# Moving the x2 low-part subtraction from GpSimd to VectorE, with a two-step longer lag

## The reference

```python
kv_pool = kv.reshape(B, H//4, 4, W//4, 4, C).mean(axis=(2, 4))      # 768 keys
k = v = kv_pool.reshape(B, -1, C) @ w_sr
x = softmax(q @ k.T / sqrt(C)) @ v                                  # attention

g = relu(x @ w_in) ** 2                                             # first MoE block, d_ff = 2048
x = g @ w_out

h = x @ w_in                                                        # second block
P = a[0] + a[1]*h + a[2]*h**2 + a[3]*h**3
Q = 1 + abs(b[0])*abs(h) + abs(b[1])*h**2
out = (P / (Q + 1e-6)) @ w_out
```

## Time and profile before

| what | value |
|---|---|
| median of 3 runs | 1538.09 us (1538.04 to 1538.12) |
| the profiled execution's own time | 1538.09 us |
| its span (first to last instruction) | 1536.2 us |
| TensorE busy | 1486.7 us, 97% |
| VectorE busy | 1441.0 us, 94% |
| ScalarE busy | 1376.9 us, 90% |
| GpSimd busy | 1186.1 us, 77% |
| mean granted TensorE clock | 0.996 of full |

### The profile page before, as it was taken

One profiled execution on the slowest core, in us unless ns is written; L12 is line 12 of the kernel. 1 busy time (PEld: TensorE's weight loads), 2 busy tenths in 40 slices (PEclk: granted clock), 3 DMA queues, 4 the chain that ended last, 5 costly groups with the idle time before them and its releaser, 6 DMA issues.

```text
span 1536.2 us, 20302 instructions
## 1 busy us (share of the span) xinstructions
PE 1486.7 (97%) x5452; PEld 966.8 (63%) x5452; DVE 1441.0 (94%) x2543; ACT 1376.9 (90%) x2605; POOL 1186.1 (77%) x1167
## 2 busy tenths in 40 slices
PE   5999999999999999999999999999999999999975
PEld 3899999755666556656656665665665665566532
DVE  7888888539999999999999999999999999999998
ACT  3777777679999999999999999999999999999985
POOL 2544444478898888888888989888988988898874
PEclk9999999999999999999999999999999999999998
DMA  6000003000000000000000000000000000000000
GB/s 220 27 22 22 26 20 109 0 0 1 8 7 8 1 8 7 8 7 1 8 8 7 1 8 8 7 1 7 8 8 7 1 8 7 7 1 8 7 7 7
DMA packets 11223, 24.39 MB, mean 16 GB/s; under 512 B 1408, under 2 KB 1536, under 8 KB 10880
## 3 DMA queue, kind: packets, MB, share of 16 engines
q1 hardware_dynamic: 11136, 23.40, 4.5%
HBM read 17.11 MB, written 6.29 MB: 15 GB/s over the span
## 4 chain that ended last, share of the span: by engine, by line
PE 80%; DVE 14%; issue 3%; ACT 1%; POOL 1%; DMA 1%; SPq 0%; POOLq 0%; ACTq 0%; DVEq 0%
PE psum L644 18%; PE psum L633 17%; PE psum L534 10%; PE psum L535 9%; PE psum L536 9%; PE psum L594 6%; PE psum L569 6%; PE psum L580 4%; DVE tb L524 3%; DVE tb L501 3%; DVE tb L507 3%; DVE psum L512 3%; DMA X<-kvT 1%; SPq L186 0%; POOL pnorm L240 0%
## 5 line engine op out<-in xcount | busy, mean ns | idle before, releaser
L292 POOL TENSOR_TENSOR wb<-wb,ub 128x512 f32<-128x512 f32 x384 | 496.6, 1293 | 32.0
L633 PE MATMUL psum<-tb,wout 128*128 128x512 f32 x768 | 396.0, 597 | 5.9 <-DVE tb L524 4.4
L644 PE MATMUL psum<-g,wout 128*128 128x512 f32 x768 | 392.6, 593 | 1.9 <-ACT x2f L380 1.0
L290 POOL TENSOR_SCALAR wb<-ub,babs 128x512 f32<-128x512 f32 x384 | 297.3, 774 | 118.0 <-ACT ub L391 118.0
L392 ACT ACTIVATE tb<-psum,ca 128x512 f32<-128x512 f32 x384 | 311.0, 810 | 0.0
L534 PE MATMUL psum<-x2h,win2h 128*128 128x512 f32 x384 | 291.4, 759 | 18.1 <-DVE tb L524 15.2
L518 DVE TENSOR_TENSOR tb<-tb,psum 128x512 f32<-128x512 f32 x384 | 260.2, 678 | 38.1 <-ACT tb L392 38.1
L501 DVE SCALAR_TENSOR_TENSOR tb<-tb,ca,psum 128x512 f32<-128x512 f32 x384 | 282.6, 736 | 1.4 <-ACT psum L413 0.8
L507 DVE SCALAR_TENSOR_TENSOR tb<-tb,ca,psum 128x512 f32<-128x512 f32 x384 | 283.5, 738 | 0.0
L512 DVE SCALAR_TENSOR_TENSOR psum<-wb,psum 128x512 f32<-128x512 f32 x384 | 263.1, 685 | 0.0
L524 DVE SCALAR_TENSOR_TENSOR tb<-psum,tb 128x512 f32<-128x512 f32 x384 | 261.4, 681 | 0.2
(11 more groups left out here) (65 smaller groups left out, 2257.6 us busy)
## 6 DMA issues: line engine op xcount, KB each, us to landing
qraw<-qT SPq DMA_DIRECT2D x25, 256.0 KB, 2.7
X<-kvT SPq DMA_DIRECT2D x16, 384.0 KB, 8.1
outT<-osb SPq DMA_DIRECT2D x24, 256.0 KB, 2.0
wraw<-w_in SPq DMA_DIRECT2D x2, 1024.0 KB, 10.8
wsr<-w_sr SPq DMA_DIRECT2D x1, 64.0 KB, 1.9
wout<-w_out SPq DMA_DIRECT2D x2, 0.5 KB, 8.1
ca<-coef_a SPq DMA_DIRECT2D x1, 2.0 KB, 2.2
cb<-coef_b SPq DMA_DIRECT2D x1, 1.0 KB, 2.1
```

The lines of the kernel that those rows point to most:

```text
L290: nc.gpsimd.tensor_scalar(w, u, babs[:, 1:2], babs[:, 0:1], ALU.mult, ALU.add).then_inc(v_rdy, 1)
L292: nc.gpsimd.tensor_tensor(w, w, u, ALU.mult).then_inc(w_rdy, 1)
L633: mm(ACC2, wout2[:, f, :], tb[:, t % T_RING, :], start=(f == 0), stop=(f == NF - 1))\
L644: mm(ACC1, wout1[:, f, :], g1[:, t % G_RING, :], start=(f == 0), stop=(f == NF - 1))\
```

## The change

- The copy x2f, its buffer and its semaphore go. GpSimd's subtraction goes.
- VectorE subtracts x2h straight from ACC1 to give x2l, as the first thing in its step 16c + 18, in front of that step's five operations. It waits for x2h_rdy.
- TensorE's first ACC1 matmul of the next chunk now waits for x2_rdy (x2l is there).
- LAG is NF + 5 in place of NF + 3: the second block follows two steps later, and the loop has two steps more.
- On TensorE ACC1 comes before ACC2 within a step. On ScalarE the x2h copy comes before osb, and the square of an even slice is issued one step later (t = s - 2).

```diff
-    LAG = NF + 3
+    LAG = NF + 5
@@ GpSimd
-                t = s - 3
-                if chunk_end(t):
-                    c = t // NF
-                    pool.wait_ge(x2h_rdy, c + 1)
-                    pool.wait_ge(x2f_rdy, c + 1)
-                    nc.gpsimd.tensor_tensor(x2l[:, c % 2, :], x2f[:, c % 2, :], x2h[:, c % 2, :].bitcast(F32),
-                                            ALU.subtract).then_inc(x2_rdy, 1)
@@ ScalarE
+                t = s - 3
+                if chunk_end(t):
+                    c = t // NF
+                    act.wait_ge(g1_used, t + 1)
+                    need(act, h2_rdy, (c - 1) * NF)
+                    nc.scalar.activation(x2h[:, c % 2, :], ACC1, ACT.Identity).then_inc(x2h_rdy, 1)
+
                 t = s - LAG - 5
                 if chunk_end(t):
                     ...
                     nc.scalar.activation(osb[:, c % 2, :], ACC2, ACT.Copy, scale=-1.0).then_inc(o_rdy, 1)
 
-                t = s - 3
-                if chunk_end(t):
-                    c = t // NF
-                    act.wait_ge(g1_used, t + 1)
-                    need(act, h2_rdy, (c - 1) * NF)
-                    nc.scalar.activation(x2h[:, c % 2, :], ACC1, ACT.Identity).then_inc(x2h_rdy, 1)
-                    need(act, x2_rdy, c - 1)
-                    nc.scalar.activation(x2f[:, c % 2, :], ACC1, ACT.Identity).then_inc(x2f_rdy, 1)
-
-                t = s - 1
+                t = s - 2
                 if in_b(t) and on_act(t):
@@ VectorE
             for s in range(STEPS):
+                t = s - 3
+                if chunk_end(t):
+                    c = t // NF
+                    dve.wait_ge(x2h_rdy, c + 1)
+                    nc.vector.tensor_tensor(x2l[:, c % 2, :], ACC1, x2h[:, c % 2, :].bitcast(F32),
+                                            ALU.subtract).then_inc(x2_rdy, 1)
+
                 t = s - LAG - 2
@@ TensorE
+                t = s - 2
+                if in_b(t):
+                    f = t % NF
+                    if t == 0:
+                        pe.wait_ge(x_rdy, NCH)
+                    if f == 0:
+                        need(pe, x2_rdy, t // NF)
+                    pe.wait_ge(sqa_rdy if on_act(t) else sqp_rdy, t // 2 + 1)
+                    mm(ACC1, wout1[:, f, :], g1[:, t % G_RING, :], start=(f == 0), stop=(f == NF - 1))\
+                        .then_inc(g1_used, 1)
+
                 t = s - LAG - 4
                 ...
-                t = s - 2
-                if in_b(t):
-                    ...
-                    if f == 0:
-                        need(pe, x2f_rdy, t // NF)
-                    ...
```

More of the change, by code:

```diff
@@ L104, in build_program @@
         osb = sb("osb", [P, 2, T], F32, atB)
-        x2f = sb("x2f", [P, 2, T], F32, atB)
         psum = ctx.enter_context(nc.psum_tensor("psum", [P, 8, BANK], F32))
@@ L138, in build_program @@
             sem, ("t1_rdy", "t2_rdy", "t3_rdy", "y_rdy", "e_rdy", "g2_rdy", "g2_used", "o_rdy"))
-        x2f_rdy = sem("x2f_rdy")
         o_out = [sem("o_out0"), sem("o_out1")]
@@ L634, in _ @@
                         .then_inc(g2_used, 1)
-                t = s - 2
-                if in_b(t):
-                    f = t % NF
-                    if t == 0:
-                        pe.wait_ge(x_rdy, NCH)
-                    if f == 0:
-                        need(pe, x2f_rdy, t // NF)
-                    pe.wait_ge(sqa_rdy if on_act(t) else sqp_rdy, t // 2 + 1)
-                    mm(ACC1, wout1[:, f, :], g1[:, t % G_RING, :], start=(f == 0), stop=(f == NF - 1))\
-                        .then_inc(g1_used, 1)
 def kernel(q, kv, w_sr, moe_w_in, moe_w_out, moe2_w_in, moe2_w_out, moe2_a, moe2_b):
```

## The result

The changed kernel takes 1553.01 us (median of four runs, 1552.72 to 1554.16) against 1538.11 us for the kernel before in the same comparison: a ratio of 1.0097, 95% interval 1.0085 to 1.0109. That is 14.9 us slower; the forecast was 14.8. The profiled execution took 1553.61 us, with a span of 1551.4, 15.2 more than before.

What follows compares the result with a forecast made beforehand. VectorE at its 3.11 us step floor, with TensorE equally close, was taken to bound the kernel; 13.8 - 3.8 + 1.3 + 2.7 + 0.8 = +14.8 us on 1538.1 gave 1552.9, predicted 1553, range 1549 to 1558.5.

Steps and rivals of the forecast that it cites:

- VectorE's step of 3.11 us is its floor: VectorE's five operations per step: 3.11 us in tail and middle alike, so added work adds to the time.
- The subtraction at 0.60 us, less 3.8 us of idle time: VectorE at chunk boundaries: 23 subtractions of 0.60 us cost 13.8 us, less 3.8 us of idle time absorbed.
- The hand-over: Chunk boundary: VectorE waits 0 to 0.1 us for x2h; TensorE's step becomes 3.68 us in place of 3.11.
- The term for the two engines' small difference: Chunk boundaries: 0.06 us a chunk for the engines' difference and an occasional late Exp or square, 1.3 us in all.
- LAG + 2: Start of the second stage: two more first-stage steps of 1.56 us make the first H2 and L501 2.7 us later.
- The very start: Loop start: first square moves behind a ReLU and a weight split on ScalarE; 0.8 us, bounds 0 and 1.2.
- "Cost nothing" for the square: ScalarE's square one step later: ends 0.08 us before the weight load that needs it, so no cost.
- Rival A: Square or x2h comes late in ordinary steps: 5.5 us more, 1558.4 us; chance 0.16.
- Rival B: The two extra steps are free and the start loses nothing: +10.0, 1548.1 us; chance 0.06.
- Rival C: 3.11 us isn't VectorE's floor, a step could take 3.07 and hide the subtraction: 1539.3 us; chance 0.04.
- Rival D: The subtraction on VectorE takes 0.65 us in place of 0.60: 1.2 us more, 1554.1 us; chance 0.06.

Runs made afterwards that it cites:

- experiment 1: The kernel before with the subtraction for x2l on VectorE alone, x2f copy gone, LAG and orders kept: 1548.05 us, ratio 1.0058.
- experiment 2: The changed kernel with a second VectorE subtraction of the same size per chunk, which releases nobody: 1566.38 us, ratio 1.0179.
- experiment 3: The kernel before with LAG = NF + 5 alone: 1539.4 us, ratio 1.0001.
- experiment 5: The changed kernel with the subtraction left out from the third chunk on and the square issued one step earlier: 1540.64 us, ratio 1.002.
- experiment 4: The changed kernel with the subtraction left out from the third chunk on, x2h alone releasing TensorE: 1549.55 us, ratio 1.0069.
- experiment 8: The kernel before with idle VectorE making win2l's four parts and the first chunk's x2l ahead of its loop: 1536.38 us, ratio 0.9992.
- experiment 10: The kernel before with both the start's subtractions on idle VectorE and the later wait for x2l: 1535.08 us, ratio 0.998.
- experiment 9: The kernel before with a chunk's first H2 waiting for x2h alone, only its last product waiting for x2l: 1536.25 us, ratio 0.9989.

## Why the prediction was right, point by point

- **VectorE's step of 3.11 us is its floor.** Right. L497 is still 3.11 us apart inside a chunk, and an additional operation costs itself (experiments 1 and 2).
- **The subtraction at 0.60 us, less 3.8 us of idle time.** Right: experiment 1 isolates the two, and they make 10.0 us. The source given for the idle time was wrong, though: the two ScalarE copies ahead of the Exp. With both copies and no wait of TensorE for x2l (experiment 3) VectorE idles 1193.7 - 1191.0 = 2.7 us; with one copy fewer (experiment 5, one subtraction of 0.6 taken off) still 1194.0 - 0.6 - 1191.0 = 2.4. TensorE's 16 undisturbed steps of 3.120 us are 0.15 longer than VectorE's 49.77, and that alone makes up to 3.3 us in 22 chunks. The copies only set the step in which VectorE catches up and waits.
- **The hand-over.** x2h, the subtraction and TensorE's step of 3.67 us came out to a few hundredths. The term for the two engines' small difference was 1.3 us; the steps grew by 10.9 - 10.0 = 0.9. In the changed kernel one VectorE interval per chunk is 3.71 to 3.81, as predicted. The part above 3.71 is VectorE's wait for x2h, up to 0.1 us.
- **LAG + 2.** From the last accumulation before the boundary, 324.28 before and 325.80 after, the gap to L501's first start grew from 9.74 to 12.48 us: 2.7, as predicted.
- **The very start.** Mis-sized. 4.3 us were lost before VectorE's first step, where 3.5 were forecast. 325.80 less 324.28 is 1.5 us, of which 0.16 were there at the first H1 already (297.13 before, 297.29 after), so the square's move took about 1.4 us in place of 0.8, which also lies above the upper bound of 1.2. Experiments 4 and 5 give 1.3 for it. The rows of the changed kernel (start, duration):

```profile
299.90 0.62 ACT L375 ACTIVATE g<-r 128x512 f32<-128x512 f32 x1
300.63 0.30 PEld L631 LDWEIGHTS psum<-g,wout 128*128 128x128 f32 x2 [1.18 <-issue]
300.66 1.10 PE L631 MATMUL psum<-g,wout 128*128 128x512 f32 x2 [0.78 <-ACT g L375]
...
304.19 0.30 PEld L631 LDWEIGHTS psum<-g,wout 128*128 128x128 f32 x2 [0.61 <-ACT g L375]
304.19 0.70 PE L631 MATMUL psum<-g,wout 128*128 128x512 f32 x1 [0.17 <-ACT g L375]
```

  The first square costs about the 0.8 us (0.78 in the row; counted from the first H1 the accumulation starts 0.9 us later than before). The second even slice meets the same weight split again, at 304.19, and adds 0.3; that one was left out of the estimate. The errors, +0.8 at the start (0.2 of it from phase A) and -0.4 in the steps, partly cancelled. That the medians agree with the forecast to 0.1 us is in part luck.
- **"Cost nothing" for the square.** Right for ordinary steps: between 500 and 1400 us the load waits for it 13 times, 2.1 us in all, 0.2 at most. Incomplete for the boundary: the square stands behind x2h there, and by itself it would cost TensorE 0.4 us a chunk if the subtraction weren't later still (experiments 4 and 5). The prediction didn't name that cover. On this point the sum was right by luck: a longer wait lay over the square's.
- **Rival A** (late hand-overs, 1558) did not come: no ordinary step grew. **Rival B** (start for free) is refuted by 338.3, although in experiment 3, where the subtraction is absent, the longer lag does pay back 1.1 of its 2.5 us at the boundaries. **Rival C** (VectorE has room) is refuted by experiments 1 and 2. **Rival D** (0.65 to 0.66 us): 0.61 between starts at the boundary shown, and 0.60 in the trace of experiment 2. The Trainium skill's row for a PSUM source (VectorE: DVE Perf Modes, section on the TRN2 errata) gives an estimate of 658 ns. The subtraction at 0.60 to 0.61 us from start to start doesn't bear that out, and the measurement decides.
- The Trainium skill says that taking work off a saturated VectorE may make sense (Perfetto Trace Analysis, section Optimizing Scalar/DVE Operations). Experiment 1, which does the reverse, agrees with it: 10.0 us more in VectorE's steps. Experiments 8 and 10 add that the same kind of subtraction costs nothing on VectorE in a stretch in which it idles.

## What to carry to other kernels

When two engines show the same busy share, measure each one's floor from start to start, where the other is out of the way (here the tail), before moving work between them; then the price of an added instruction can be written down to the tenth. Behind every wait stands the next one: to price a removed wait, follow what else is queued in front of the same reader, at the boundary step and not only in an ordinary one. Count the loop's first steps separately, since a change of order that is free in the steady state can cost at a start where other work shares the engine. And compare starts of two profiles from an event that the change can't touch.

## What the runs showed of the hardware that was not expected

- TensorE's ordinary step has two lengths, 3.113 and 3.120 us, and keeps one over many steps (before: 16 steps in 49.91 or 50.01 us, boundary included). The same instructions run in both, and the granted clock from 500 to 1400 us is 1.00 of full speed. Over a chunk that is 0.1 us, as much as the waits that experiments 9 and 10 removed. Before, about half of the chunks had the short step; in experiment 3, where those waits are gone, 346 of the 347 steps from the second chunk to the tail have the long one. Its cause is open.
- In experiment 8 two of the four weight subtractions on VectorE, which read two SBUF tensors, took 1.21 and 1.12 us; the other two took 0.68 and 0.69. The two long ones had started while a GpSimd product of 1.04 us was running, and ended 0.55 us after it. The rows (the VectorE rows hold two subtractions each):

```profile
299.68 1.04 POOL L298 TENSOR_TENSOR g<-r 128x512 f32<-128x512 f32 x1 [7.74 <-ACT r L405]
300.06 1.81 DVE L497 TENSOR_TENSOR win2l<-wraw,win2h 128x512 fp32r<-128x512 f32 x2 [7.49 <-ACT win2h L343]
...
302.12 1.04 POOL L298 TENSOR_TENSOR g<-r 128x512 f32<-128x512 f32 x1 [1.39 <-ACT r L405]
302.59 1.89 DVE L497 TENSOR_TENSOR win2l<-wraw,win2h 128x512 fp32r<-128x512 f32 x2 [0.72 <-ACT win2h L343]
```

  The subtraction out of PSUM in the changed kernel (L490) took 0.671 to 0.692 us all 24 times, with GpSimd 75% busy. The Trainium skill (SBUF — State Buffer, section SBUF: two separate sides) says that a VectorE instruction with two SBUF inputs and a GpSimd one that reads SBUF exclude each other: the one that starts first blocks the other for its whole length. These four rows agree with it. It speaks for reading ACC1 from PSUM rather than a copy of it in SBUF.
- In experiment 2 it is GpSimd that waits. The added subtraction reads the same SBUF tile twice, and each time it takes its usual 0.68 us (0.75 once); the GpSimd operation w that runs beside it takes 1.30 to 1.36 us in 21 chunks, where the 361 that don't meet it take 0.76 to 0.79. So the same tile read twice behaves as two SBUF inputs here. One pair of rows:

```profile
780.62 0.68 DVE L493 TENSOR_TENSOR x2s<-x2h 128x512 f32<-128x512 f32 x1
...
780.65 1.30 POOL L282 TENSOR_SCALAR wb<-ub,babs 128x512 f32<-128x512 f32 x1 [0.54 <-ACT ub L381]
```

  GpSimd isn't the bottleneck, and the chunk grew by VectorE's 0.60 us and no more.
